# x1 tiles laid 16 and 48 bytes behind the weights' place modulo 64, and two products no longer read by turns

## The reference, cut to what matters

```python
def attention(q, k, v, alpha):                 # 4 batches, 8 heads, 768 steps, 48 numbers a head
    for t in range(S):
        state = alpha[:, :, t, :, None] * state + einsum('bhd,bhe->bhde', k[:, :, t], v[:, :, t])
        y[:, :, t] = einsum('bhd,bhde->bhe', q[:, :, t], state)
def bilinear(x, w1, w2, w3, w_out):            # 3072 tokens, 384 -> 1024 -> 384
    return ((x @ w1) * (x @ w2)) @ w3 @ w_out
def experts(x, probs, w1, w2):                 # 4 experts, 384 -> 1024 -> 384, all of them for every token
    p = probs / (probs.sum(-1, keepdims=True) + 1e-09)
    return sum(p[:, e:e+1] * (maximum(x @ w1[e], 0) @ w2[e]) for e in range(4))
```

## Time and profile before

| | us |
|---|---|
| median of three runs | 1204.76 (1203.73 to 1204.92) |
| the profiled execution, its own time | 1204.63 |
| its span, first to last instruction | 1202.9 |
| TensorE matmul busy | 1197.2 (100%) |
| TensorE weight loads busy | 1038.9 (86%) |
| VectorE, ScalarE, GpSimd busy | 549.5, 287.2, 161.2 |
| granted TensorE clock, mean | 1.000 of full |

### The profile page before, as it was taken

How to read it: one execution, slowest core, us unless ns; L and a number is a source line. 1 busy time by engine, 2 the same in 40 slices (tenths; PEclk the granted TensorE clock), 3 DMA queues, 4 the chain that set the end, 5 groups by cost and what they waited for, 6 DMA issues and landing times.

```text
span 1202.9 us, 17638 instructions
## 1 busy us (share of the span) xinstructions
PE 1197.2 (100%) x7164; PEld 1038.9 (86%) x7164; DVE 549.5 (46%) x1008; ACT 287.2 (24%) x527; POOL 161.2 (13%) x147
## 2 busy tenths in 40 slices
PE   9999999999999999999999999999999999999998
PEld 8799999999999988888888888888888888888887
DVE  6997686676751112222234434433434344344333
ACT  3443333332323411111111211112112112111111
POOL 1132222222222500000000000000000000000000
PEclk9999999999999999999999999999999999999999
DMA  9644543543613370011151111115011111222201
GB/s 300 198 125 105 146 128 89 164 125 74 164 48 138 119 301 25 28 52 53 53 210 53 53 52 52 53 53 201 21 41 52 53 53 53 79 79 78 78 1 52
DMA packets 89782, 114.34 MB, mean 95 GB/s; under 512 B 39152, under 2 KB 57968, under 8 KB 88688
## 3 DMA queue, kind: packets, MB, share of 16 engines
q1 hardware_dynamic: 89424, 112.97, 29.7%
q10 hardware_dynamic: 288, 0.39, 0.1%
HBM read 92.59 MB, written 18.40 MB: 92 GB/s over the span
## 4 chain that ended last, share of the span: by engine, by line
PE 98%; DMA 1%; DVE 1%; SPq 0%; ACT 0%; issue 0%; DVEq 0%; ACTq 0%
PE bank L1225 33%; PE bank L1342 22%; PE score_banks L1342 11%; PE bank L1069 9%; PE bank L1071 9%; PE bank L1070 9%; PE bank L1110 2%; PE bank L1293 1%; PE score_banks L1131 1%; PE bank L1120 1%; PE score_banks L1094 1%; DMA wo_sb<-w_out 1%; DVE total L1029 0%; PE bank L1078 0%; DVE w_lo L924 0%; DVE suffix L768 0%
## 5 line engine op out<-in xcount | busy, mean ns | idle before, releaser
L1225 PE MATMUL bank<-x_lo,we_hi 128*128 128x512 f32 x576 | 224.2, 389 | 0.0
L1225 PE MATMUL bank<-x_hi,we_lo 128*128 128x512 f32 x576 | 224.1, 389 | 0.0
L1225 PE MATMUL bank<-x_hi,we_hi 128*128 128x512 f32 x576 | 224.1, 389 | 0.0
L1037 DVE SCALAR_TENSOR_TENSOR h_scaled<-bank,gate_rows 128x512 f32<-128x512 f32 (+1 forms) x145 | 99.5, 687 | 246.1 <-PE bank L1225 246.0
L732 ACT ACTIVATE h_hi<-h_scaled 128x512 fp32r<-128x512 f32 (+1 forms) x145 | 91.2, 629 | 484.5 <-DVE h_scaled L1037 484.5
L1342 PE MATMUL bank<-h_hi,we_hi 128*128 128x512 f32 x384 | 149.5, 389 | 0.0
L1342 PE MATMUL bank<-h_hi,we_lo 128*128 128x512 f32 x384 | 149.4, 389 | 0.0
L1342 PE MATMUL bank<-h_lo,we_hi 128*128 128x512 f32 x384 | 149.4, 389 | 0.0
L1041 DVE TENSOR_TENSOR h_lo<-h_scaled,h_hi 128x512 fp32r<-128x512 f32 (+1 forms) x145 | 99.9, 690 | 100.1 <-ACT h_hi L732 100.1
L518 POOL TENSOR_TENSOR we_lo<-we_raw,we_hi (+1 forms) x48 | 61.0, 1291 | 535.6 <-ACT we_hi L579 535.6
L1069 PE MATMUL bank<-x,wb_hi 128*128 128x384 f32 x384 | 128.6, 335 | 0.0
(11 more groups left out here) (103 smaller groups left out, 1655.8 us busy)
## 6 DMA issues: line engine op xcount, KB each, us to landing
x_hi<-x_hi_spill SPq DMA_DIRECT2D x24, 768.0 KB, 4.9
x_lo<-x_lo_spill SPq DMA_DIRECT2D x24, 768.0 KB, 6.4
we_raw<-wset SPq DMA_DIRECT2D x4, 3072.0 KB, 10.5
inputs<-akq SPq DMA_DIRECT2D x24, 448.0 KB, 5.1
values<-v_rows SPq DMA_DIRECT2D x24, 256.0 KB, 3.5
gate_rows<-gate_spill SPq DMA_DIRECT2D x4, 1536.0 KB, 13.8
inputs<-akq SPq DMA_DIRECT2D x24, 224.0 KB, 3.3
x_hi_spill<-x_hi_out SPq DMA_DIRECT2D x8, 576.0 KB, 4.3
```

Source lines behind the costliest of these rows:

```text
L1037: dve.scalar_tensor_tensor(out=h_scaled[:, s % 2, part], in0=bank[s % 2][:, part], scalar=0.0, in1=gate_rows[e % 2][:, at], op0=ALU.max, o ...
L1225: mm = pe.matmul(dst, (we_hi if term < 2 else we_lo)[e % 2][:, cols], moving, start=(i == 0), stop=(i == KT * TERMS - 1))
```

## The change

The two products by turns go back to plain order. Each x1 tile's buffer becomes 128 columns longer (512 bytes, so the buffers' starts keep their place modulo 512), and the tile is the part of it that begins 4 columns (16 bytes) in for the even slot and 12 columns (48 bytes) in for the odd slot. `attention_rest` shrinks by the same amount, so nothing behind it moves. The tile of x1 thus begins 16 or 48 bytes behind the place of the weights modulo 64; h stays at the weights' place. No instruction is added, taken away or moved on any engine.

```diff
-BY_TURNS = {(0, s, 4): 4 for s in (3, FT + 1)}
...
 X1_GAP = 72
-ATTENTION_REST = ATTENTION_COLUMNS - 4 * KT * TILE2 - X1_GAP
+X1_SHIFT = [4, 12]
+ATTENTION_REST = ATTENTION_COLUMNS - 4 * (KT * TILE2 + P) - X1_GAP
...
         sb("x1_gap", [P, X1_GAP])
         for slot in range(2):
-            x1_hi[slot] = sb(f"x1_{slot}_hi", [P, KT, TILE2], F32R)
-            x1_lo[slot] = sb(f"x1_{slot}_lo", [P, KT, TILE2], F32R)
+            shifted = slice(X1_SHIFT[slot], X1_SHIFT[slot] + KT * TILE2)
+            x1_hi[slot] = sb(f"x1_{slot}_hi", [P, KT * TILE2 + P], F32R)[:, shifted].rearrange("p (k t) -> p k t", k=KT)
+            x1_lo[slot] = sb(f"x1_{slot}_lo", [P, KT * TILE2 + P], F32R)[:, shifted].rearrange("p (k t) -> p k t", k=KT)
...
-                dst, moving = bank[s % 2][:, :], (x1_lo if term == 1 else x1_hi)[u][:, k, :]
-                if (e, s, i) in BY_TURNS:
-                    dst, moving = [a.rearrange("p (h a r) -> p a h r", h=2, r=BY_TURNS[e, s, i]) for a in (dst, moving)]
-                mm = pe.matmul(dst, (we_hi if term < 2 else we_lo)[e % 2][:, cols], moving, start=(i == 0), stop=(i == KT * TERMS - 1))
+                mm = pe.matmul(bank[s % 2][:, :], (we_hi if term < 2 else we_lo)[e % 2][:, cols], (x1_lo if term == 1 else x1_hi)[u][:, k, :],
+                               start=(i == 0), stop=(i == KT * TERMS - 1))
```

## The result

| | before | after |
|---|---|---|
| median of four executions, us | 1204.24 (1203.55 to 1204.92) | 1223.93 (1223.47 to 1225.17) |
| span of the profiled execution, us | 1202.9 | 1222.4 |

The change makes the kernel slower: ratio 1.0163, 95% interval 1.0151 to 1.0175, which is 19.7 us. The forecast was 1201.6 us with a range of 1190 to 1216; the result lies beyond the range.

The account below looks back on a forecast made before the run. The prediction took TensorE's matmul distances from start to start as the bound. From the profiled 1204.63 us, -2.9 (shift of x1) and -0.24 (no turns) gave 1201.5, with the median 0.13 higher 1201.6 us; range 1190 to 1216.

Parts of the forecast that it names:

- What bounds the kernel: Second stage, experts' up and down matmuls: TensorE never idle at full clock, so only the 226.74 ns from start to start counts.
- Loads of x1, longer buffers, first stage: Shifted x1 loads stay hidden, longer buffers add no instruction or wait, first stage still ends at 413.9 us: cost nothing.
- the cover of eight steps: An x1 tile is wanted some eight steps (32.6 us) after its load's issue, hiding the 6.4 us landing.
- Products by turns, -0.24 us: Experts' up products: six by turns each cost 0.04 us with the three products behind; plain order saves 0.24 us.
- The shift of x1, -2.9 us: Up products: starting x1 off the weights' place removes one meeting of 1.67 ns in each of 1728; down products unchanged.
- left-over of 13.3 ns: Time per product beyond one column per cycle at 2.4 GHz, the same for 384 and 512 columns.
- eight equal meetings modulo 64: Moving tile overtakes the weight load's place modulo 64 bytes eight times per product, 1.67 ns (four columns) each.
- the sign that its mechanism is wrong: Distance after down products, whose operands all stay where they lay, changing as well; forecast kept it at 226.7 ns.
- Rival 3: Experts' products lose the regular pattern: +8.5 us in up products alone (1213.0), +16.9 in both (1221.4); 28 in 100.
- Rival 1: Experts' pattern doesn't depend on x1's start; only the products by turns save time, 1204.5 us; 28 in 100.
- Rival 2: Most of the up products' left-over goes: half gives 1193.0 us, all 1181.5; 14 in 100.

Follow-up runs that it names:

- e1: The kernel after the change with both x1 tiles back at the weights' place, still without products by turns; 1204.32 us, ratio 1.0001 to the kernel before.
- e4: The kernel after the change, with even x1 tiles 64 bytes and odd ones 4 bytes behind the weights' place; 1228.55 us.
- e5: The kernel after the change, with even x1 tiles 128 bytes and odd ones 512 bytes behind the weights' place; 1210.17 us.
- e8: The kernel after the change, with even x1 tiles 256 bytes and odd ones 480 bytes behind the weights' place; 1209.96 us.
- e9: The kernel after the change, with a 32-byte pad ahead of all tensors, even x1 tiles at the weights' place, odd ones 224 bytes behind; 1210.08 us.
- e13: The kernel after the change, x1 at the weights' place; in even tiles seven of nine up products load 64 of 128 weight columns; 1211.79 us.
- e6: The kernel after the change, with h 16 bytes behind the weights, even x1 tiles at the weights' place, odd ones 16 bytes behind; 1220.87 us.
- e2: The kernel after the change with the two products by turns put back, shifts of 16 and 48 bytes kept; 1224.15 us, ratio 1.0163.

## Why the prediction was wrong

- **What bounds the kernel**: right. Distance from start to start, no waits, no other engine; 5.74 ns x 3427 is the whole change.
- **Loads of x1, longer buffers, first stage**: right at nothing; landing 6.4 us as before, the experts begin within 0.2 us of where they did. (The 32.6 us from load to load are those from 803.84 to 836.48, and the two slots take turns, so each slot is loaded every 65 us; the cover of eight steps is as the prediction has it.)
- **Products by turns, -0.24 us**: right, by e1's trace.
- **The shift of x1, -2.9 us: this is the step that failed.** "I take one fewer, since a meeting at the start is the one that a shift of either sign moves" gave -1.7 ns for each up product and nothing for the down products. Measured are +5.0 ns for each product in even and +6.7 ns in odd tiles, +19.7 us in all: the up distance grew by 1.7 and 7.5 ns, the down distance by 8.3 and 5.8. The prediction had named a changed distance after the down products as the sign that its mechanism is wrong, and that sign is there. Two assumptions went wrong. I turned a left-over of 13.3 ns into eight equal meetings modulo 64, though no row showed either number: the period is 256 bytes (e4, e5, e8, e9), and products with half the load take longer, not less (e13). And I costed the shift on the products that stream x1 alone, where the regular 226.7 ns was a property of the sequence: in e6 shifting h takes the same 5.0 ns from the pair as shifting x1 does. The 1.67 ns of a meeting, the time of four columns, do fit most of the measured means, which lie whole steps apart (226.7, 230.0, 231.7, 233.3, 236.7, 240.0). But 230.8 ns at 64 bytes does not fit, nor do the means of the half loads, and since the eight meetings behind the number have fallen, the fit is no support for them. The sign and the count were wrong.
- **Rival 3 is what came true**, with its full price: up and down products both, 1221.4 us, against 1223.9. Its rows, the lone products, were the only ones that priced the loss of the pattern. (Their 231.6 ns was read from rounded starts; at full resolution they take 231.2, which gives 1220.3 us.) That the price came so near is in part luck: with x1 16 bytes off, the lone products themselves take 230.5 ns ((415.57 - 413.73) / 8 in the rows after the change, by rounded starts 230), 0.7 ns **less** than before, while the products that take turns went to 231.7. e1 has 231.2 and e2 230.5 ns again. So the lone products are another sequence with its own order of places (in e4, at 64 bytes, they take 230.2), and what they cost says nothing certain about what a shift costs the others. Rival 3's mechanism is half right: the pattern does go, but the ones that replace it are regular, between 226 and 236 ns, and hold until the tile changes. My argument against it, that each disturbance was over within four products, spoke of disturbances that pass; a changed place stays. The range left that price out with 11 chances in 100.
- **Rival 1 and the rule of two read ports.** In these runs a matmul's distance depends on where it reads against where the weights are read: 226.7 ns at 0 and 240.0 ns at 240 bytes, and 226.7 again when all are moved together (e9). By the rule in the Trainium skill, "TensorE: Matmul & The Clock Gate", section "Step-by-step: what each phase is for", that loading the next weights takes no read bandwidth from the running matmul, the two places could not matter. Here, for float32r products of 512 columns, they do, and the measurement decides. Whether it is bandwidth that they share, no run shows.
- **Rival 2** never showed: no place gave a mean below 226.7 ns, 13.3 over the bare columns. The 225.0 ns of the up products at 192 bytes is paid back by the down products.

**What stays open.** Why 4, 208 or 240 bytes are worse than 96 or 128, why 192 is as good as 0 for x1 or h alone and not for both, why 32 bytes hold two patterns, and why a half load at the weights' place costs 4.4 ns, is measured and not explained. The runs show that the relative place modulo 256 acts, that the read order of the moving tile acts and the order of its writes does not, that a product with half the load takes part in another pattern, and that all this falls on the sequence and not on one product alone. They show no mechanism.

## What to carry to other kernels

Where TensorE is never idle and the clock is full, read the distance from start to start of like products; if it is longer than the columns take, the places of the moving tile and of the weights against each other are a parameter, worth up to 6% of the distance here, and it can be swept with a pad and slack in the buffers, two places to a run by giving two buffers of a double buffer different shifts. Read more than one round of each, since one place can hold two patterns. Begin with all operands of the matmuls at the same place modulo 256 bytes; here none of 13 other places modulo 256 was better for products that take turns. For up products alone, 16 and 64 bytes were slightly better (230.5 and 230.2 ns against 231.2), so sweep with the sequence that the kernel has. And when a regular pattern is what you have, price its loss on all the products that take part in it.

## What the runs showed of the hardware that was not expected

- The distance of float32r matmuls of 512 columns depends on the moving tile's place against the weights, period 256 bytes, between 226.7 ns (0, 192) and 240.0 ns (240). Moving all operands together by 32 bytes changes nothing.
- One place can hold two patterns: 32 bytes behind, 230.0 ns in the round entered from lone products and 231.7 in the eleven entered from the other tile.
- Up products without down products between them order the places otherwise: 231.2 ns at 0, 230.5 at 16, 230.2 at 64.
- 4 bytes of shift cost more (236.7 ns) than 16 or 32 (231.7).
- Most mean distances lie whole steps of 1.67 ns above 226.7 (230.0, 231.7, 233.3, 236.7, 240.0); 230.8 at 64 bytes does not.
- A moving tile read by turns in runs of 16 bytes from two halves 1024 bytes apart takes 256.7 ns at the weights' place, 30 more than in plain order there, and adds 10 ns to the down product behind it; at 32, 128 and 192 bytes it takes 238.3, 252.5 and 239.1 ns. Writing PSUM by turns costs nothing (226.7).
- Loading 64 weight columns in place of 128, and so writing 64 PSUM partitions, lengthened the mean distance from 226.7 to 231.1 ns at the weights' place, and shortened it from 231.7 to 228.9 and from 233.3 to 230.7 ns at the change's places.
